# Softmax probabilities scaled on GpSimd ahead of their transpose, in place of a transposed tile of reciprocals after the product with V

## The reference, cut to what matters

```python
scores = scale * q @ k.T                       # B=2, H=8 heads, S=768, D=64
keep = (pos_k < n_sink) | (0 <= pos_q - pos_k < window)      # 4 sinks, window 128
scores = where(keep, scores, -1e9); scores -= scores.max(-1)
a = exp(scores)
a = a / (a.sum(-1) + 1e-9)                     # the part that the change touches
x = (a @ v) as (1536 tokens, 512)
g = x @ w_gate;  x = (silu(g) * (x @ w_val)) @ w_out          # dense layer, d_ff 1536
# then a skip test per token, a top-1 router over 8 experts, and
# out = x + gate * (relu(x @ w1[e]) @ w2[e]) for the tokens kept
```

## Time and profile before

| What | us |
|---|---|
| median of 3 runs | 569.79 (568.99 to 569.99) |
| the profiled execution's own time | 567.21 |
| its span, first to last instruction | 565.6 |
| PE busy | 546.5 (97%) |
| DVE busy | 243.5 (43%) |
| ACT busy | 180.9 (32%) |
| POOL busy | 97.4 (17%) |
| attention stage on PE, first scores to the first product of the dense layer | 6.49 to 87.66 |

### The profile page before, as it was taken

The page is one execution under the profiler, slowest core; times in us unless marked ns, Lnnn a source line. Parts: engine busy times, 40 slices in busy tenths (PEclk is TensorE's granted clock), DMA queues, the critical chain, the costliest instruction groups (busy, mean ns, idle before and its releaser), DMA issues.

```text
span 565.6 us, 10760 instructions
## 1 busy us (share of the span) xinstructions
PE 546.5 (97%) x3837; PEld 462.7 (82%) x3837; DVE 243.5 (43%) x686; ACT 180.9 (32%) x421; POOL 97.4 (17%) x137
## 2 busy tenths in 40 slices
PE   7899999999999999999999999999889999999994
PEld 5677777888888888888888888888779999999993
DVE  6777762323233233332432344633641452455151
ACT  5677862221202212121133424322411331343140
POOL 2234457201111100100000010010211111111111
PEclk9999999999999999999999999999999999999998
DMA  8988532110111111000063112761376598396211
GB/s 218 256 269 245 163 100 71 65 30 25 56 56 56 56 56 55 0 0 1 0 231 122 46 54 76 267 264 56 103 250 265 194 364 316 124 343 214 83 38 37
DMA packets 29591, 73.84 MB, mean 131 GB/s; under 512 B 2832, under 2 KB 15120, under 8 KB 25456
## 3 DMA queue, kind: packets, MB, share of 16 engines
q1 hardware_dynamic: 26592, 63.61, 33.3%
q0 software_dynamic: 2960, 9.73, 5.1%
HBM read 62.03 MB, written 11.29 MB: 130 GB/s over the span
## 4 chain that ended last, share of the span: by engine, by line
PE 92%; DVE 2%; DMA 2%; issue 2%; POOL 1%; ACT 1%; POOLq 0%; DVEq 0%
PE bank L1485 13%; PE bank L1280 12%; PE bank L1282 12%; PE bank L1284 12%; PE bank L1357 6%; PE bank L1361 6%; PE bank L1359 6%; PE bank L1266 4%; PE bank L1497 4%; PE bank L1499 4%; PE bank L1498 4%; PE bank L1243 3%; PE bank L1222 3%; PE bank L1377 2%; PE bank L1236 1%
## 5 line engine op out<-in xcount | busy, mean ns | idle before, releaser
L1280 PE MATMUL bank<-x_hi,w_hi 128*128 128x512 f32 x288 | 112.2, 390 | 0.5 <-issue 0.5
L1284 PE MATMUL bank<-x_hi,w_lo 128*128 128x512 f32 x288 | 112.1, 389 | 0.0
L1282 PE MATMUL bank<-x_lo,w_hi 128*128 128x512 f32 x288 | 112.0, 389 | 0.0
L1485 PEld LDWEIGHTS bank<-xgT,w_sb 128*128 128x128 f32 x704 | 80.2, 192 | 1.9 <-issue 1.1
L1485 PE MATMUL bank<-xgT,w_sb 128*128 128x128 f32 x704 | 80.5, 275 | 0.9 <-ACT xgT L802 0.9
L998 DVE TENSOR_TENSOR sig<-sig,bank 128x512 f32<-128x512 f32 x36 | 24.8, 688 | 127.2 <-ACT sig L704 127.2
L704 ACT ACTIVATE sig<-bank 128x512 f32<-128x512 f32 x36 | 21.5, 598 | 159.7 <-PE bank L1284 159.7
L1280 PEld LDWEIGHTS bank<-x_hi,w_hi 128*128 128x128 f32 x288 | 54.1, 188 | 12.0 <-issue 0.9
L1284 PEld LDWEIGHTS bank<-x_hi,w_lo 128*128 128x128 f32 x288 | 54.1, 188 | 11.3
L1282 PEld LDWEIGHTS bank<-x_lo,w_hi 128*128 128x128 f32 x288 | 54.1, 188 | 11.1
L1357 PE MATMUL bank<-wo_hi,hh_hi 128*128 128x512 f32 x132 | 53.6, 406 | 0.0
(11 more groups left out here) (169 smaller groups left out, 757.4 us busy)
## 6 DMA issues: line engine op xcount, KB each, us to landing
w_raw<-w SPq DMA_DIRECT2D x16, 1024.0 KB, 6.8
w_sb<-w SPq DMA_DIRECT2D x16, 1024.0 KB, 8.4
w_raw<-w_gv SPq DMA_DIRECT2D x12, 512.0 KB, 3.5
va_sb<-v_long SPq DMA_DIRECT2D x10, 512.0 KB, 3.6
vb_sb<-v_tail SPq DMA_DIRECT2D x10, 320.0 KB, 4.7
xg<-expert_rows POOLq DMA_DIRECT2D x12, 257.0 KB, 3.0
q_sb<-qT SPq DMA_DIRECT2D x12, 256.0 KB, 5.0
k_sb<-kT SPq DMA_DIRECT2D x12, 256.0 KB, 6.1
```

The source lines that it names most:

```text
L1280: nc.tensor.matmul(ps[:, :], w_hi[:, u, a, k, :], x_hi[:, k, tok], start=(k == 0), stop=False)
L1282: nc.tensor.matmul(ps[:, :], w_hi[:, u, a, k, :], x_lo[:, k, tok], start=False, stop=False)
L1284: last = nc.tensor.matmul(ps[:, :], w_lo[:, u, a, k, :], x_hi[:, k, tok], start=False, stop=(k == KD - 1))
L1485: last = nc.tensor.matmul(ps, w1_sb[u][:, k, fc], xgT[:, k * P:k * P + P], start=(k == 0), stop=(k == KD - 1))
```

## The change

The division by the sum moves from after the product with V to before the transpose.

- POOL multiplies the probabilities of each head by that head's reciprocal, in place in `probs` (8 instructions a tile, 128x208 or 128x128). `rsum_wide`, `rbc_sb` and `xT` are gone, and with them R on PE and ACT, and POOL's `split_x`.
- Q comes once for two pairs (four heads), in the round after their S, ahead of X. T of a pair waits for `probs_scaled` and is done for pairs g-4 and g-3; V for pairs g-6 and g-5. X is for a tile's last pair 8 or 7 back.
- X: ACT makes `x_hi` straight from PSUM, then DVE makes `x_lo` from PSUM and `x_hi`.
- POOL's `split_w` goes in halves behind the scalings of tiles 9 to 11, and its work on `w_out` waits for the last V.
- `find_wide` moves from round 6 to round 24.

```diff
-def on_act(kind, h):
-    return kind == "R" or h == HP - 1
+def on_act(n):
+    return n % HP == HP - 1
...
         for n in (g, g + 1):
             if n < PAIRS:
                 steps.append(("S", n // HP, n % HP, n))
-        for n in (g - 7, g - 6):
+        if 0 <= g - 2 < PAIRS:
+            steps.append(("Q", (g - 2) // HP, (g - 2) % HP, (g - 2) // 2))
+        for n in (g - 8, g - 7):
             if 0 <= n < PAIRS and n % HP == HP - 1:
                 steps.append(("X", n // HP, None, n // HP))
-        for n in (g - 3, g - 2):
+        for n in (g - 4, g - 3):
             if 0 <= n < PAIRS:
-                steps.append(("T", n // HP, n % HP, psum_use))
...
-                if n % HP == HP - 1:
-                    steps.append(("Q", n // HP, None, n // HP))
-        for n in (g - 5, g - 4):
+                steps.append(("T", n // HP, n % HP, n))
+        for n in (g - 6, g - 5):
             if 0 <= n < PAIRS:
                 tile, hp = divmod(n, HP)
-                steps.append(("V", tile, hp, None))
-                if hp == HP - 1:
-                    steps.append(("R", tile, None, psum_use))
-                    psum_use += 1
+                steps.append(("V", tile, hp, n))
                 if tile in EARLY and hp == 1:
                     steps.append(("W", tile, None, tile - EARLY[0]))
         if g in MASK_AT:
             steps.append(("K", MASK_AT[g], None, g))
+        if g == PAIRS // 2:
+            steps.append(("F", 0, None, g))
...
 POOL:
-            for tile in range(NT):
-                if tile == QT - 1:
+            for i in range(PAIRS // 2):
+                tile, first = divmod(i * 2, HP)
+                qt = tile % QT
+                if tile == QT - 1 and first:
                     copy_sinks(1)
-                pool.wait_ge(rsum_ready, tile + 1)
-                nc.gpsimd.tensor_copy(rsum_wide.rearrange("p (h c) -> p h c", h=H),
-                                      rsum[:, tile % 2, :].unsqueeze(2).broadcast_to([P, H, D])).then_inc(rsum_spread, 1)
-                if tile:
-                    split_x(tile - 1)
-                    if tile - 1 in EARLY:
-                        split_w(tile - 1 - EARLY[0])
-            split_x(NT - 1)
-
+                pool.wait_ge(rsum_ready, i + 1)
+                cols = slice(0, SC if qt else P)
+                for h in range(first * 2, first * 2 + 4):
+                    last = nc.gpsimd.tensor_scalar(probs[:, qt % 2, h, cols], probs[:, qt % 2, h, cols],
+                                                   rsum[:, tile % 2, h:h + 1], None, ALU.mult)
+                    if h % 2:
+                        last.then_inc(probs_scaled, 1)
+                early = tile - 2 - EARLY[0]
+                if early in range(len(EARLY)):
+                    half_k = slice(0, KD // 2) if first == 0 else slice(KD // 2, KD)
+                    last = split_w(early, half_k)
+                    if first:
+                        last.then_inc(w_lo_made, 1)
+            for n in range(NT - 2 - EARLY[0], len(EARLY)):
+                split_w(n, slice(0, KD)).then_inc(w_lo_made, 1)
+
+            pool.wait_ge(pv_done, PAIRS)
...
 ACT:
-                elif kind == "R":
-                    a.wait_ge(pT_in_psum, n + 1)
-                    if tile:
-                        a.wait_ge(o_ready, tile)
-                    nc.scalar.activation(rbc_sb, pT_ps[n % 2][:, :], ACT.Copy).then_inc(pT_by_act, 1)
+                elif kind == "X":
+                    a.wait_ge(pv_done, tile * HP + HP)
+                    nc.scalar.activation(x_hi[:, :, tile * P:tile * P + P], o_ps[tile % 2][:, :].rearrange(
+                        "p (k t) -> p k t", k=KD), ACT.Copy).then_inc(x_hi_made, 1)
...
 DVE:
                 elif kind == "Q":
-                    d.wait_ge(probs_ready, tile * H + H)
-                    nc.vector.tensor_scalar(rsum[:, tile % 2, :], sums[:, qt % 2, :], 1e-9, None, ALU.add
+                    heads = slice(h * 2, h * 2 + 4)
+                    d.wait_ge(probs_ready, n * 4 + 4)
+                    if n >= 4:
+                        d.wait_ge(probs_scaled, n * 2 - 6)
+                    nc.vector.tensor_scalar(rsum[:, tile % 2, heads], sums[:, qt % 2, heads], 1e-9, None, ALU.add
                                             ).then_inc(sums_step, 1)
...
                 elif kind == "X":
-                    use = next(m for k, t, _, m in ORDER if k == "R" and t == tile)
-                    d.wait_ge(pv_done, LAST_V[tile] + 1)
-                    d.wait_ge(pT_by_act, evacuated(use)[1])
-                    if tile >= 2:
-
-                        d.wait_ge(xT_ready, tile - 1)
-                    nc.vector.tensor_tensor(xT[:, tile % 2, :], o_ps[tile % 2][:, :], rbc_sb, ALU.mult
-                                            ).then_inc(o_ready, 1)
+                    d.wait_ge(x_hi_made, tile + 1)
+                    at_tok = slice(tile * P, tile * P + P)
+                    nc.vector.tensor_tensor(x_lo[:, :, at_tok], o_ps[tile % 2][:, :].rearrange("p (k t) -> p k t", k=KD),
+                                            x_hi[:, :, at_tok].bitcast(F32), ALU.subtract).then_inc(xT_ready, 1)
                 elif kind == "K":
                     make_mask(tile)
-                    if tile == 0:
-                        find_wide()
+                elif kind == "F":
+                    find_wide()
...
 PE, T:
-                        pe.wait_ge(probs_ready, tile * H + h * 2 + 2)
+                    pe.wait_ge(probs_scaled, n + 1)
...
 PE, first V of a tile:
-                            pe.wait_ge(o_ready, tile - 1)
+                            pe.wait_ge(xT_ready, tile - 1)
```

More of the change, by code:

```diff
@@ L47 @@
 WARM_UP = 24
-def on_act(kind, h):
-    return kind == "R" or h == HP - 1
+def on_act(n):
+    return n % HP == HP - 1
 def attention_order():
-    steps, psum_use, turned = [], 0, {}
+    steps = []
     for g in range(0, PAIRS + 10, 2):
@@ L85, in attention_order, with evacuated @@
             steps.append(("K", MASK_AT[g], None, g))
[L86 to L100, removed]
+        if g == PAIRS // 2:
+            steps.append(("F", 0, None, g))
+    return steps
+ORDER = attention_order()
+def evacuated(n):
+    engine = on_act(n)
+    return engine, sum(on_act(m) == engine for m in range(n + 1))
 def build(nc, qT, kT, v, va, vb, sizes, w_gv, w_out, w_route, w1, w2, out):
@@ L386, in load_values @@
                 if tile >= 3:
-                    sp.wait_ge(pv_done, LAST_V[tile - 3] + 1)
+                    sp.wait_ge(pv_done, (tile - 2) * HP)
                 if t == 0:
@@ L531, in _ @@
             pool.sem_inc(idx_copied, DONE)
[L532 to L539, removed]
             def copy_sinks(b):
@@ L908, in _ @@
                             accum_out=negmax[:, i % 4:i % 4 + 1]).then_inc(max_ready, 1)
-                elif kind == "T" and not on_act(kind, h):
+                elif kind == "T" and not on_act(n):
                     d.wait_ge(pT_in_psum, n + 1)
-                    if SBUF_USE[n] >= TURNED:
-                        d.wait_ge(pv_done, SBUF_USE[n] - TURNED + 1)
-                    nc.vector.tensor_copy(turned(probsT[:, SBUF_USE[n] % TURNED, :], qt), turned(pT_ps[n % 2][:, :], qt)
+                    if n >= TURNED:
+                        d.wait_ge(pv_done, n - TURNED + 1)
+                    nc.vector.tensor_copy(turned(probsT[:, n % TURNED, :], qt), turned(pT_ps[n % 2][:, :], qt)
@@ L918, in _ @@
                                             ).then_inc(sums_step, 1)
-                    d.wait_ge(sums_step, tile + 1)
-                    nc.vector.reciprocal(rsum[:, tile % 2, :], rsum[:, tile % 2, :]).then_inc(rsum_ready, 1)
+                    d.wait_ge(sums_step, n + 1)
+                    nc.vector.reciprocal(rsum[:, tile % 2, heads], rsum[:, tile % 2, heads]).then_inc(rsum_ready, 1)
                 elif kind == "X":
-                    use = next(m for k, t, _, m in ORDER if k == "R" and t == tile)
@@ L1227, in step @@
                                     last.then_inc(scores_ready, 1)
-                elif kind in "TR":
+                elif kind == "T":
                     if n >= 2:
@@ L1232, in step @@
                         pe.wait_ge(pT_by_act if by_act else pT_by_dve, count)
-                    if kind == "R":
-                        pe.wait_ge(rsum_spread, tile + 1)
-                        for hp in range(HP):
-                            last = nc.tensor.transpose(pT_ps[n % 2][:, hp * P:hp * P + P],
-                                                       rsum_wide[:, hp * P:hp * P + P], ident[:, :])
-                    else:
-                        pe.wait_ge(probs_ready, tile * H + h * 2 + 2)
-                        for u in range(2):
-                            for at, width in ((0, P), (P, TAIL))[:2 if qt else 1]:
-                                to = u * 2 * P + at
-                                last = nc.tensor.transpose(pT_ps[n % 2][0:width, to:to + P],
```

(9 more changed lines are left out.)

23 lines of the change are left out of this document (8 added, 15 removed).

## The result

The changed kernel takes 583.52 us (median of 6 runs, 582.49 to 586.01) against 569.84 for the kernel before, measured beside it: ratio 1.0247, interval 1.0226 to 1.0269. The forecast was 571.8 and a range up to 574.5. The direction was right and the size far off: 13.7 us in place of 2.0. The profiled execution takes 583.69 us, its span is 582.1.

What follows compares the result with a forecast made beforehand. PE bounded the kernel before (6.73 us a tile); afterwards the wait for `x_hi` would set 6.93. The profiled 567.21 + 2.0 gave 569.2, and the median's 2.58 above it gave 571.8, range 569.0 to 574.5.

Steps and rivals of the forecast that it cites:

- the term of GpSimd's scaling: One POOL scaling in attention takes 0.36 us, ends 0.30 and 1.28, and costs nothing under PE's other work.
- The threshold: Both rounds of a tile fit while one POOL scaling takes under 0.72 us; at 0.74, well under 1 us in all.
- the wait for `x_hi`: In B rounds DVE's `x_lo` waits for ACT's `x_hi` behind four exps: 6.93 us a tile against 6.73.
- the start: First attention rounds, bound by DVE: round 10 comes 1.93 us earlier, round 14 1.93 less 0.20, near 24.6.
- The split of weights fits as well: POOL's weight halves, about 0.7 us behind each four scalings in tiles 9 to 11, fit in the rounds.
- The rival that happened: POOL becomes the bound from 0.72 us a scaling; at 1.0, 8.0 us a tile and 583 in all; chance 0.04.
- The removal of R: On PE in attention, R costs 0.80 us a tile, 9.6 us in all, which surely leaves PE.
- the middle with `find_wide`: Rounds 22 to 34, narrow tile: 0.59 of `find_wide`'s 0.90 us is on the path; round 34 starts 0.28 late.
- The change touches nothing there: After 87.66 us, PE's part behind attention starts later or earlier and keeps its length.
- a different length after the first product: Sign that the forecast is wrong: the part after the first dense product changes length.

Runs made afterwards that it cites:

- the kernel with the code moved: Changed kernel plus eight never-executed transposes (16 instructions) at the head of PE's general-case branch: 578.57 us, ratio 1.0166.
- the copy experiment: Changed kernel with GpSimd's scaling replaced by a copy of each head's probabilities onto themselves, division left out: attention stage 83.38 us against 91.64.
- the scalings shared: Changed kernel with ACT doing `x_hi` ahead of the exps and the last of each four scalings, PE's code moved by 16 instructions: 567.25 us, ratio 0.9968.
- the kernel with `x_hi` first alone: Changed kernel with ACT doing `x_hi` ahead of the exps and PE's code moved by 16 instructions, all scalings on GpSimd: 579.16 us in one run.

## Why the prediction was wrong

**The step that failed** is the term of GpSimd's scaling: "I take 0.36, one tensor being read". It measured 0.80 by mean, 0.786 from one to the next. The price came from copies, and an arithmetic operation had no row of its own. The nearest row of arithmetic was the one with two inputs, at about 0.6, and even that was too low. The rule cited from the Trainium skill (GPSIMD Engine Reference, Engine selection: near line rate for one input) doesn't hold for this operation: the rows show 2.45 ns a column, three times a copy's, and the measurement decides.

**The threshold was soft too.** The forecast put the point at 0.72 and said that a little over it would cost "well under 1 us in all". The scaling at 0.80, or 0.79 from one to the next, cost 8.3 more than the copy. What was missed is first that past the point the lateness doesn't stay in one round: it comes back through a loop. There are two such loops, of nearly the same length:

- Over one tile, without `x_hi`: scalings of a B round, T, V, scores, row minima, Q, scalings of the next B round. The chain that ended last takes this one from 26.59 to 41.32 in the changed kernel, 7.29 and 7.44 a tile.
- Over two tiles, with `x_hi`: from the end of a B round's scalings at 33.73 to `x_lo` at 39.00 is 5.27, to the next scaling at 41.85 is 2.85, then come twice 3.14, in all 14.40, or 7.20 a tile. In the kernel with the code moved the chain goes through `x_hi` at 25.42 and 32.64, and a tile takes 7.21.

That is why taking the wait for `x_hi` out of the second changed nothing: the first stood ready at 7.21. Q ahead of the row minima, with the addition left out, shortens both, and only then does GpSimd's own work bound the tile, at 6.24 with all eight scalings.

Steady tiles are the smaller part, though: 1.8 of the 8.3 us between rounds 14 and 34. Also missed were the start, where four narrow scalings take 2.4 us while PE has nothing else and its clock falls after them (round 14 came at 28.23, or 27.5 counted from the first scores of before; 24.6 was forecast), and tiles 9 to 11, where 3.14 + 0.73 = 3.87 of GpSimd stand in each round: the stage lost 6.2 us after round 34, of which 1.7 were forecast. "The split of weights fits as well" was wrong for that reason.

**The rival that happened** was named, with its engine and roughly its point, and given 0.04. It deserved far more, since its only guard was a price read off another kind of operation; the bounds 0.30 to 1.28 put most of their width on its side. That its 583 is so near the measured 583.52 is luck: it was the sum for a scaling of 1.0 and a tile of 8.0 us, and 5 us of the measured time lie behind the stage.

**What was right.** The removal of R, the wait for `x_hi`, its price (6.93 a tile), the start and the middle with `find_wide`: the copy experiment shows each to within some 0.6 us (the start the worst: 1.1 us gained by round 14 where 1.7 were forecast). The forecast sum was right for a kernel whose scaling costs what a copy does.

**What was not in it at all:** 5.0 us behind the stage, from where PE's code comes to lie, about a third of the result. "The change touches nothing there" was true of the instructions and false of their place. The forecast did name a different length after the first product as a sign that it was wrong.

**Still open:** why an arithmetic operation with one input costs 2.45 ns a column on GpSimd, why VectorE's addition runs beside one part of a scaling and not the rest, and what PE waits for after the jump.

## What to carry to other kernels

Price an operation from a row of the same operation on the same engine; when there is none, let the range and the rival's chance reach to where its dearer neighbours would put it. When an engine takes over a step inside a loop of waits, compare its work per round with the round, not only with the slack, because past that point lateness goes round: here taking away the wait for `x_hi` gave nothing while the scaling was dear, and 11.7 us once it was cheap. Compare such an edit with the kernel that differs in it alone; against the changed kernel it seemed to gain 0.1 to 0.2 us a tile. An operation that starts another engine's work (Q here) belongs at the head of its round as soon as its inputs are from an earlier one; with the scalings shared, that and leaving out the addition turned 567.3 us into 559.7.

## What the runs showed of the hardware

- GpSimd, fp32, 208 columns: 0.36 us for a copy, 0.73 for a multiplication with an immediate, 0.80 with a pointer. ACT's copy with a scale took 0.45.
- GpSimd's arithmetic with one input costs about as much a column as with two: 2.45 ns (0.61 us for 128 columns, 0.80 for 208) against 2.15 (0.73 for 256, 1.28 for 512).
- VectorE's `tensor_scalar` on 128x4 sums in SBUF took 0.17 to 0.94 us. Beside scalings of 208 columns it ended with the scaling when it began 0.43 us or more after that one's start, and took 0.16 to 0.17 when it began 0.30 to 0.37 after it. The reciprocal on the same sums always took 0.17 to 0.18.
- After a jump PE stood idle for 2.6 to 4.2 us without a semaphore in the six kernels with PE's code as the change left it. In the six with 16 instructions more in the part jumped over it was idle for 0.2 to 0.6 us at the jump itself and no more.
- PE's granted clock fell to 0.50 at the end of the 3.80 us of idle time. It fell also in the start of the changed kernel (0.52 from 13.4 to 16.8 us), after PE had idled for 1.01 and 0.72 us within 2 us, and in the kernel with `x_hi` first alone, at 92.9 us, after PE had idled for 0.90 and 0.93 us within 3 us.
